# Fourier matmuls placed between the heads of a chunked recurrence, masked scores in two buffers, signs on ScalarE

## The reference

```python
# q, k, v, a_re, a_im: (4, 8, 768, 48); a gated linear recurrence with complex decay
mag = np.sqrt(a_re * a_re + a_im * a_im)
scale = np.minimum(mag, 0.999) / (mag + 1e-06)
...
for t in range(S):
    S_re, S_im = ar * S_re - ai * S_im + kv, ar * S_im + ai * S_re   # kv = k_t outer v_t
    y[:, :, t] = einsum('bhd,bhde->bhe', q[:, :, t], S_re)
# x = y as (4, 768, 384)
X = np.fft.fft(np.fft.fft(x, axis=1), axis=2)
u = x + np.real(X)
un = (u - mean(u)) / np.sqrt(var(u) + 1e-06)
x = u + np.maximum(un @ w_ch1, 0) @ w_ch2
# then a token-mixing and a channel-mixing layer
```

## Time and profile before

| | us |
|---|---|
| median of 3 runs | 1138.62 (1131.98 to 1141.57) |
| profiled execution | 1134.15 |
| its span in the trace | 1132.4 |
| of it up to the last addition of the Fourier transform | 419.4 |
| granted TensorE clock, mean over the span | 0.928 of full speed |

### The profile page before, as it was taken

How to read it: one execution, slowest core, us unless ns; L and a number is a source line. 1 busy time by engine, 2 the same in 40 slices (tenths; PEclk the granted TensorE clock), 3 DMA queues, 4 the chain that set the end, 5 groups by cost and what they waited for, 6 DMA issues and landing times. The chain is left out here.

```text
span 1132.4 us, 15567 instructions
## 1 busy us (share of the span) xinstructions
PE 1008.8 (89%) x6082; PEld 971.8 (86%) x6082; DVE 538.2 (48%) x1040; ACT 341.4 (30%) x515; POOL 29.9 (3%) x15
## 2 busy tenths in 40 slices
PE   0469799989969973999999999968999999999998
PEld 0348699979969863999999999968999999999998
DVE  6798877897973338332432422225223322331411
ACT  6636545655621113121122112124121220310310
POOL 0000000000000004000000000004000000000000
PEclk9859759779969895999999999999999999999999
DMA  4559777765757013602102101001001000100000
GB/s 151 150 152 301 221 226 224 208 196 156 196 145 281 22 44 100 223 29 84 33 22 69 42 28 63 15 23 43 15 8 46 24 14 21 42 21 15 6 22 21
DMA packets 96887, 104.79 MB, mean 93 GB/s; under 512 B 13121, under 2 KB 90433, under 8 KB 96834
## 3 DMA queue, kind: packets, MB, share of 16 engines
q1 hardware_dynamic: 96834, 104.07, 29.7%
HBM read 70.93 MB, written 33.11 MB: 92 GB/s over the span
## 5 line engine op out<-in xcount | busy, mean ns | idle before, releaser
L1125 ACT ACTIVATE hh<-mbank 128x384 fp32r<-128x384 f32 x192 | 94.5, 492 | 370.8 <-PE mbank L1309 370.8
L1218 DVE SCALAR_TENSOR_TENSOR hl<-mbank,hh 128x384 fp32r<-128x384 f32 x192 | 107.1, 558 | 200.9 <-ACT hh L1125 200.9
L1307 PE MATMUL mbank<-nTh,w1h 128*128 128x384 f32 x576 | 193.9, 337 | 0.7 <-DVE w1l L1240 0.7
L1308 PE MATMUL mbank<-nTl,w1h 128*128 128x384 f32 x576 | 193.2, 335 | 0.0
L1309 PE MATMUL mbank<-nTh,w1l 128*128 128x384 f32 x576 | 193.2, 335 | 0.0
L1307 PE MATMUL mbank<-w2h,hh 128*128 128x384 f32 x576 | 193.1, 335 | 0.0
L1309 PE MATMUL mbank<-w2h,hl 128*128 128x384 f32 x576 | 192.4, 334 | 0.0
L1308 PE MATMUL mbank<-w2l,hh 128*128 128x384 f32 x576 | 192.4, 334 | 0.0
L1307 PEld LDWEIGHTS mbank<-nTh,w1h 128*128 128x128 f32 x576 | 108.8, 189 | 1.5 <-issue 1.3
L1308 PEld LDWEIGHTS mbank<-nTl,w1h 128*128 128x128 f32 x576 | 108.8, 189 | 0.0
L1309 PEld LDWEIGHTS mbank<-nTh,w1l 128*128 128x128 f32 x576 | 108.7, 189 | 0.0
(11 more groups left out here) (152 smaller groups left out, 1320.7 us busy)
## 6 DMA issues: line engine op xcount, KB each, us to landing
kT<-k_turn SPq DMA_DIRECT2D x24, 384.0 KB, 3.6
qT<-q_turn SPq DMA_DIRECT2D x24, 384.0 KB, 4.4
q_turn<-w_raw SPq DMA_DIRECT2D x30, 192.0 KB, 4.4
k_turn<-t SPq DMA_DIRECT2D x24, 192.0 KB, 4.0
k_turn<-w_early SPq DMA_DIRECT2D x24, 192.0 KB, 4.6
u_scratch<-y_sb SPq DMA_DIRECT2D x24, 192.0 KB, 3.1
w_raw<-in_moe_w_ch SPq DMA_DIRECT2D x2, 2304.0 KB, 10.3
x_early<-u_scratch SPq DMA_DIRECT2D x4, 1152.0 KB, 10.0
```

The source lines that it names most:

```text
L1125: nc.scalar.activation(hh[:, m, :], mm_bank[(g * (KF + TPG) + m) % 2][:, 0:TG], ACT.Relu).then_inc(h_high, 1)
L1218: nc.vector.scalar_tensor_tensor(out=hl[:, m, :], in0=mm_bank[(g * (KF + TPG) + m) % 2][:, 0:TG], scalar=0.0, in1=hh[:, m, :].bitcast(fp32 ...
L1307: nc.tensor.matmul(out, lh, rh, start=(n == 0), stop=False)
L1308: nc.tensor.matmul(out, lh, rl, start=False, stop=False)
```

## The change

- **PE.** `middle`, `width_transform` and `sequence_transform` no longer stand at the ends of chunks. `fourier_beside(m, h)` is called after each head: in j = 0 the middle and the third part of the width transform, in j = 1 its other two parts, in j = 2 to 5 a quarter each of the 42 sequence matmuls. In the first block it issues one matmul of 193 columns per head instead of `keep_busy(3)` per chunk. Tiles share two PSUM banks in another order (`tile_bank`, `sums_freeing`): tiles 2 and 3 both use the bank of tile 0.
- **Masked scores.** `pr` has two buffers, by the parity of m; `masked(m, half)` waits for the outputs of m-2 and is issued in two halves with gate steps between them. `output` waits for its half alone.
- **Signs.** The two comparisons on DVE (L473, L491) become a Sign and an Identity on ACT behind each Arctan; the result of the second stands in `t4`, which `magnitudes` shares, so that one waits for the phases of the parts before.
- **DVE.** The running minimum (two small instructions per part) becomes one reduction at the end. `products` of the second and third chunk of a part and two pairs of `add_transform` are issued as single instructions of double width. `logs` is split: its two first instructions stand ahead of the first mask, its scans between the masks. The fold is done by thirds of the sequence.
- **ACT.** `keys_turned` and `evacuate_y` move ahead of the squares, magnitudes, inverses and factors.
- **SP.** The loads of the third part's q and k and of the fourth part's gates move ahead of the first `turn_decay`; `turn_over` of a part's second chunk moves one chunk later; each transform's store moves with its addition.
- **Start and end.** The first part's chain on ACT and DVE runs ahead of the second's. Behind chunk 23 the middle and a third of the width transform run ahead of the last turn.

```diff
+        PAIRS = [[range(0, 1), range(1, 3)] if p.chunks == 3 else [range(p.chunks)] for p in parts]
-        pr = sb("pr", [P, H, P])
+        pr = sb("pr", [P, 2, H, P])
...
+        def sums_freeing(b, i):
+            return b * NT + (i - 1 if b == B - 1 else (0, 0, 1, 3, 3, 4)[i])
...
@@ sync
             turn_over(0)
+            load_qk(p2)
+            load_gates(p3)
             turn_decay(p0)
-            load_gates(p3)
-            load_qk(p2)
...
@@ scalar, arctangents
                 A(t3_b[s][:, :, T], t3_b[s][:, :, T], ACT.Arctan).then_inc(act_step[s], 1)
+                A(im_b[p.r][:, :, T], re_b[p.r][:, :, T], ACT.Sign, scale=3.0,
+                  bias=nearly_zero[:, 0:1]).then_inc(act_step[s], 1)
+                act.wait_ge(act_step[s], act0[p.n] + 12)
+                A(t4[:, :, angles_room(p)], im_b[p.r][:, :, T], ACT.Identity, scale=-0.25,
+                  bias=quarter[:, 0:1]).then_inc(act_step[s], 1)
...
@@ vector, one chunk
-                for n, i in added_at(m):
-                    add_transform(n, i)
-                if b and j == 1:
-                    fold_sequence(b - 1)
                 if (m, 3) in stage_at:
-                    phases(stage_at[m, 3])
+                    half_angles(stage_at[m, 3])
+                    phases(stage_at[m, 3], range(2))
...
+                if (m, 1) in stage_at:
+                    logs(stage_at[m, 1])
...
-                masked(m)
+                masked(m, 0)
+                if (m, 3) in stage_at:
+                    phases(stage_at[m, 3], range(2, 3))
                 if (m, 0) in stage_at:
                     squared(stage_at[m, 0])
                 if (m, 1) in stage_at:
-                    logs(stage_at[m, 1])
+                    log_sums(stage_at[m, 1])
                 if (m, 2) in stage_at:
                     ends(stage_at[m, 2])
                     tangents(stage_at[m, 2])
                     scaled(stage_at[m, 2])
+                masked(m, 1)
+                for n, i, tiles in added_at(m):
+                    add_transform(n, i, tiles)
+                for n, third in folded_at(m):
+                    fold_sequence(n, third)
...
@@ tensor
+            def fourier_beside(m, h):
+                b, t = m // NCH - 1, m % NCH
+                if b < 0:
+                    mm(f_bank[0][:, 0:FH], ident[:, :], fold[:, 0, 0, 0:FH], start=True, stop=True)
+                elif t == 0:
+                    if h == 1:
+                        middle(b)
+                    if h in (5, 7):
+                        width_transform(b, 2, h // 7)
+                elif t == 1:
+                    if h % 2:
+                        width_transform(b, 1 - h // 4, h % 4 // 2)
+                else:
+                    first, end = (SEQ * NT * (8 * (t - 2) + h + n) // (4 * H) for n in range(2))
+                    for step in range(first, end):
+                        sequence_transform(b, step // SEQ, [step % SEQ])
```

More of the change, by code:

```diff
@@ L249, in _ @@
                     turn_decay(stage_at[m, 4])
-                for n, i in added_at(m - 1):
-                    store_u(n, i)
+                for n, i, tiles in added_at(m - 1):
+                    for tile in range(i, i + tiles):
+                        store_u(n, tile)
                 if m % 3 == 1:
@@ L279, in _ @@
                     sp.dma_start(w2_early, w2_next.rearrange("(k p) n -> p k n", p=P)).then_inc(w_fetched, 16)
-            for n, i in added_at(NM - 1):
-                store_u(n, i)
-            store_u(B - 2, 5)
+            for n, i, tiles in added_at(NM - 1):
+                for tile in range(i, i + tiles):
+                    store_u(n, tile)
             for i in range(NT):
@@ L310, in magnitudes @@
                 A(t3_b[s][:, :, T], t1_b[s][:, :, T], ACT.Exp, scale=0.5).then_inc(act_step[s], 1)
-                if p.n:
-                    act.wait_ge(vec_step[1 - s], vec0[p.n - 1] + 3)
-                A(t4[:, :, T], re_b[p.r][:, :, T], ACT.Abs).then_inc(act_step[s], 1)
+                for o in parts[max(p.n - 2, 0):p.n] if p.n > 1 else []:
+                    act.wait_ge(vec_step[o.s], vec0[o.n] + 7 + 3 * o.chunks)
+                A(t4[:, :, angles_room(p)], re_b[p.r][:, :, T], ACT.Abs).then_inc(act_step[s], 1)
             def inverses(p):
@@ L426, in _ @@
             evacuate_y(NM - 1)
+            middle(B - 1)
+            widths(B - 1, 2)
             y_turned(NM - 1)
-            middle(B - 1)
-            for n in range(KD):
-                widths(B - 1, n)
+            widths(B - 1, 1)
+            widths(B - 1, 0)
         @block.vector
@@ L673, in output @@
                 later = m % NCH > 0
[L674 removed]
+                if h % 4 == 0:
+                    pe.wait_ge(sc_free, 2 * m + h // 4 + 1)
+                made = mm(y_bank[:, cols], pr[:, m % 2, h, :], v_sb[:, p.s, m - p.first, cols], start=True, stop=not later)
                 if later:
@@ L783, in _ @@
                 output(NM - 1, h)
+            middle(B - 1)
+            for part in range(2):
+                width_transform(B - 1, 2, part)
             turn_y(NM - 1)
```

307 lines of the change are left out of this document (158 added, 149 removed).

## The result

The changed kernel takes **1182.5 us** (median of 4 runs, 1175.19 to 1197.23) against 1138.86 on the same chip: ratio 1.037, 95% interval 1.0288 to 1.0452. It is slower by 3.7%; the forecast was 1135, the range 1108 to 1156. The medians hold every execution, and the ratios leave out those more than 1.5% above the fastest of their kernel; the profiled execution is such a one (1197.23 us, span 1195.2), so all its stretches together show 62.8 us more than before, of which 14.7 are its distance to the median and 4.7 that of the profiled execution before.

A forecast was written before the change was run, and what follows sets the result against it. Between chunks 6 and 18 neither DVE nor PE is full; they hand over to each other, and a loop through ACT follows. +3 +3 -10.4 -2.5 +4 = about -3, from the median 1135.5 us; range 1108 to 1156.

The forecast's parts named there:

- one half-clock stretch of +4: Clock term in the new loop: two strings of four outputs at twice the time, +4 us, ends 0 and +16.
- Rival 2: PE's clock falls in every turn of the loop, its 12.1 us chunk becoming up to 24: +20, 1152 us; chance 0.25.
- Between heads the matmuls cost the same: Spreading Fourier matmuls between heads leaves PE's full-clock sum per block at 70 to 71 us; only the spread changes.
- The loop through ACT: Chunks 6 to 18: outputs, ACT's copy and magnitudes, DVE's logarithms and masks wait in turn; two blocks 174.2 us, +3.
- the surest term: From 320.3 to 385.0 us, gates gone, PE runs 57.1 us, starting 2.8 ahead: 54.3 against 64.7, -10.4 us.
- The wait of 2.4 us for the bank of tile 3: In j = 4, tile 3's opening matmul waits for DVE's addition of tile 2, outputs behind it: +2.4 us.
- the start: Before PE begins at 34.4 us: the first part is ready 2.9 us earlier, not queued behind the second's load.
- the vanished wait for q: Third part's queries come some 12 us earlier, removing DVE's idle wait of 7.01 us before chunk 6's mask.
- the last stretch: Last block's transform after the outputs: 30.8 us against 34.4, taken as -2.5 us, between -3.6 and 0.
- DVE's busy time: In the profile after, DVE was to be busy some 25 us less.
- Rival 3: The second buffer does not act; the 50.4 us of mask waits stay, DVE savings alone give 1118 us; chance 0.06.

The follow-up runs named there:

- b_spread: Kernel before, with sequence-tile passes of chunks 2 to 5 between the heads and block 0's filler matmuls behind heads 1, 4, 7: 1170.8 us, ratio 1.031.
- a_copylate: Changed kernel, with ScalarE's copy of y again behind the magnitudes or factors, keys still turned first: 1132.5 us, ratio 0.998 to the kernel before.
- a_dveorder: Changed kernel, with DVE's order of before: both halves masked together, ahead of logarithms, factors and scaling: 1185.5 us, ratio 1.047 to the kernel before.
- st_onebuf: Changed kernel with passes in one run, ScalarE's old order, y turned ahead of the run, and one buffer of masked scores: 1108.1 us, ratio 0.975.
- a_actorder: Changed kernel, with ScalarE's old order inside a chunk (keys behind arctangents and sines, copy of y behind magnitudes or factors): 1139.6 us, ratio 1.001.
- a_solid_act: Changed kernel, with Fourier passes in one run behind the state update and ScalarE's old order: 1122.6 us, ratio 0.989 to the kernel before.
- a_solid: Changed kernel, with each chunk's Fourier passes in one run behind the state update instead of between heads: 1143.9 us, ratio 1.006.

## Why the prediction was wrong

- **The step that failed is the clock.** I took one half-clock stretch of +4, with +16 at the end, and put every chunk at full-clock durations. By the stretches above and the earlier trace rows, PE stood at half clock for 241 us up to the last addition of the transform, against 121 before: 120 us more, each of which does half a microsecond's work, so about 60 lost, of the 62.8 between the two profiled executions. By the medians of all executions it is some 80 us more and 40 lost, of 43.6. Rival 2 had the mechanism, "PE takes the place of DVE", and the sign that I gave for it, a clock below 0.86 between chunks 6 and 18, is there (0.69). Its price of 20 was less than half of the real one: I counted stretches that cost 4 to 5 us each, so last 8 to 10, and the six between 164 and 382 us lasted 10 to 41. I had given it a chance of 0.25.
- **"Between heads the matmuls cost the same"** is true at a given clock (at full clock chunks 22 and 23 take 12.2 and 9.6 us, from one turn of y to the next, for my 12.1 and 9.7) and misled me. It treats the spread as neutral, while b_spread alone costs 3.1%. That wide matmuls now stand among the outputs spoke, I said, against a low clock; the clock was lower.
- **The loop through ACT** was right in kind. I had DVE idle 2.9 before the logarithms and 1.4 before the factors; it idled 4.9 and 5.4 on average (34.1 / 7, 38.1 / 7). The two blocks took 218.1 instead of 174.2. In the second of them the steps from the mask of chunk 12 on were 18.5, 18.0, 18.7, 22.2, 17.9 and 12.7 us for my 16.7, 12.5, 13.5, 18.1, 12.5 and 13.8: both factor steps and the phase step of chunk 15 are 5 longer, because DVE stands in them for ScalarE, 6.4 us for the factors in chunk 14 and 3.3 and 2.4 us in chunk 15. Up to the mask of chunk 6 it was 164.3 for 152. I also put the loop down as a given and only priced it; that one place in ScalarE's queue is worth 45 us (a_copylate) I did not see. The forecast that DVE's wait for the magnitudes is what sets the length is not borne out: a_dveorder takes it from 34.1 to 9.8 us and gains nothing. Which wait in the loop does is open.
- **Chunks 19 to 23**, "the surest term", -10.4, came out at +4.5, again by the clock. The work was right (68.46 x 0.83 = 57 us at full clock); 23.9 us of it ran at half clock, with no wait over 0.3 us ahead.
- **The wait of 2.4 us for the bank of tile 3** in j = 4 did not appear; PE was late itself. The stall of that chunk is 4.3 us at the first mask.
- **Right, in this execution:** the start (31.7 us), the vanished wait for q, the last stretch (-3.4 for -2.5), DVE's busy time (-20.3 for -25) and ACT's (+21.0 for +20), and that the 50.4 us of the one buffer's wait go. They were no gain: with one buffer again the best order is as fast (st_onebuf). Rival 3 had said that the buffer doesn't act; the waits did go, and their worth is nil, in that order.

What stays open: whether two buffers pay when the passes stand between the heads. b_spread (one buffer) loses 3.1% to them and a_actorder against a_solid_act (two), which differ in the place of the passes alone, 1.2%, which hints at it, but other things differ. Which wait of the early copy lowers the clock is open too. And why a half-clock stretch lasts 10 us at one place of the changed kernel and 41 at another, none of these runs tells.

## What to carry to other kernels

On an in-order engine, an instruction that waits for the slowest partner belongs behind the work that is ready: the copy of y moved ahead of magnitudes and factors looked like an earlier release and cost about 45 us with the passes between the heads, and about 19 with them in a run (a_solid against a_solid_act). Price a new order at both clock levels of TensorE before believing its sum: ask at each handover of 2 us or more what the chunk would take at half clock, and whether PE then becomes the bound. And when filler matmuls make a kernel faster, the bound is the clock; then put them, as here, in a run behind the outputs that others wait for: the same twelve matmuls cost 37 us more between them.

## What the runs showed of the hardware

PE can stay at the half clock while it is busy with next to no gap: 40.64 of 40.90 us at 180.2 in the changed kernel, and 23.90 of 23.90 at 398.6, in a mix of matmuls of 48, 96, 128 and 193 columns in fp32. The Trainium skill (TensorE: Matmul & The Clock Gate, Part 1) says that the throttled clock is the default and that activity releases it; in these two stretches it was not released for 41 and 24 us of work. The fall at 398.6 came, like the one at 199 in the earlier trace rows, with no wait over 0.3 us ahead of it.
